# Last chunk of tokens kept in its own order and stored by SyncE; the first 1024 tokens sorted by themselves and gathered by index

## What is computed

```python
x   = local + block-summary attention(q, k, v)          # (1536, 512), 8 heads of 64
xn, en = x / |x|, expert_emb / |expert_emb|
logits = xn @ en.T / tau;  e = argmax(logits);  gate = softmax(logits)[e]
y[t]   = gate[t] * (relu(x[t] @ w1[e[t]]) @ w2[e[t]])   # 8 experts, 512 -> 1024 -> 512
h   = y @ w_in                                          # 512 -> 2048
g   = (a0 + a1 h + a2 h^2 + a3 h^3) / (1 + |b0||h| + |b1| h^2 + 1e-6)
out = g @ w_out                                         # 2048 -> 512, row t of out is token t
```

## Time and profile before

| | |
|---|---|
| median of 3 runs | 752.04 us |
| profiled execution | 747.03 us |
| its span, first to last instruction | 745.5 us |
| TensorE busy | 684.3 us (92%) |
| VectorE busy | 500.2 us (67%) |
| ScalarE busy | 419.7 us (56%) |
| GpSimd busy | 171.9 us (23%) |
| mean granted TensorE clock | 0.970 |

### The profile page before, as it was taken

The page is one execution under the profiler, slowest core; times in us unless marked ns, Lnnn a source line. Parts: engine busy times, 40 slices in busy tenths (PEclk is TensorE's granted clock), DMA queues, the critical chain, the costliest instruction groups (busy, mean ns, idle before and its releaser), DMA issues.

```text
span 745.5 us, 11775 instructions
## 1 busy us (share of the span) xinstructions
PE 684.3 (92%) x3397; PEld 547.3 (73%) x3397; DVE 500.2 (67%) x975; ACT 419.7 (56%) x786; POOL 171.9 (23%) x233
## 2 busy tenths in 40 slices
PE   4769999999387989999999999999999999999991
PEld 4457777777276777777888788888888888888871
DVE  7576677676557468433411637899989899898881
ACT  5445565565335577533523527777666666766650
POOL 4366999331331312111001000100000020200002
PEclk9989999999599999999999999999999999999997
DMA  8233544311698499823723440101000020100001
GB/s 295 56 93 113 135 131 109 79 47 45 212 325 252 139 308 323 276 59 105 265 84 100 142 157 15 57 0 30 15 14 1 1 71 1 42 15 1 0 1 56
DMA packets 52182, 77.75 MB, mean 104 GB/s; under 512 B 31680, under 2 KB 31696, under 8 KB 50840
## 3 DMA queue, kind: packets, MB, share of 16 engines
q1 hardware_dynamic: 43608, 51.51, 22.4%
q0 software_dynamic: 8064, 25.46, 10.3%
q10 hardware_dynamic: 448, 0.02, 0.1%
HBM read 63.50 MB, written 13.48 MB: 103 GB/s over the span
## 4 chain that ended last, share of the span: by engine, by line
PE 76%; DMA 10%; DVE 5%; ACT 3%; issue 2%; SPq 1%; POOL 1%; DVEq 1%; ACTq 0%; POOLq 0%
PE bank L1594 18%; PE bank L1609 17%; PE bank L1562 10%; PE bank L1341 10%; PE bank L1541 8%; DMA raw_late<-in_moe_w_dram 8%; PE bank L1450 4%; PE bank L1424 4%; PE bank L1449 3%; DVE weights L1206 2%; ACT weights L792 2%; DMA kraw<-in_k_dram 2%; PE bank L1469 1%; PE bank L1357 1%; DMA x_by_slot<-VA,zidx 1%
## 5 line engine op out<-in xcount | busy, mean ns | idle before, releaser
L1609 PE MATMUL bank<-weights,G 128*128 128x512 f32 x576 | 140.7, 393 | 1.9 <-DVE G L1206 1.9
L1594 PE MATMUL bank<-X2T,weights 128*128 128x512 f32 x576 | 141.1, 394 | 0.0
L1609 PEld LDWEIGHTS bank<-weights,G 128*128 128x128 f32 x576 | 108.1, 188 | 27.1 <-DVE G L1206 2.6
L1594 PEld LDWEIGHTS bank<-X2T,weights 128*128 128x128 f32 x576 | 107.5, 188 | 23.6
L1541 PE MATMUL bank<-weights,XT 128*128 (+1 forms) x456 | 116.9, 406 | 8.2 <-issue 4.0
L1562 PE MATMUL bank<-weights,HT 128*128 x456 | 112.6, 403 | 6.0 <-DVE HT L1206 6.0
L1541 PEld LDWEIGHTS bank<-weights,XT 128*128 128x128 f32 x456 | 85.3, 192 | 30.4 <-issue 11.8
L1562 PEld LDWEIGHTS bank<-weights,HT 128*128 128x128 f32 x456 | 85.7, 191 | 26.4 <-issue 7.1
L844 ACT ACTIVATE qd<-bank,coef 128x512 f32<-128x512 f32 x48 | 33.1, 689 | 73.5 <-PE bank L1594 73.4
L1206 DVE TENSOR_TENSOR HT<-bank,HT 128x512 fp32r<-128x512 f32 x38 | 24.5, 685 | 70.2 <-ACT HT L869 68.5
L742 ACT ACTIVATE es<-es,nmx 128x182 f32<-128x182 f32 x96 | 42.5, 444 | 25.5 <-DVE nmx L1015 25.5
(11 more groups left out here) (215 smaller groups left out, 1156.1 us busy)
## 6 DMA issues: line engine op xcount, KB each, us to landing
raw_early<-in_moe_w_dram SPq DMA_DIRECT2D x14, 1024.0 KB, 8.2
raw_late<-in_moe_w_dram SPq DMA_DIRECT2D x14, 1024.0 KB, 10.3
y_in_order<-yo POOLq DMA_DIRECT2D x19, 256.0 KB, 3.2
x_all<-in_moe_w_dram POOLq DMA_DIRECT2D x8, 512.0 KB, 3.9
kraw<-in_k_dram SPq DMA_DIRECT2D x3, 1024.0 KB, 8.3
qraw<-in_q_dram SPq DMA_DIRECT2D x12, 256.0 KB, 4.1
x<-y_in_order POOLq DMA_DIRECT2D x12, 256.0 KB, 3.1
VA<-in_v_dram SPq DMA_DIRECT2D x10, 208.0 KB
```

What stands on the lines that cost most here:

```text
L1594: last = T_.matmul(bank[6 + f % 2][:, :], W[:, 0, wa, kc * F2 + f * P:kc * F2 + (f + 1) * P], X2T[c % 2][:, xa, kc * C_TOK:(kc + 1) * C_TO ...
L1609: last = T_.matmul(bank[tt][:, :], G[:, f % 2, ga, tt * P:(tt + 1) * P], W[:, 1, wa, f * DM:(f + 1) * DM], start=(f == 0 and n_ == 0), sto ...
```

## The change

Only the first 1024 tokens (8 tiles, `SORTED`) take part in the sorting for stage C. The rows of `y_in_order` stay where they are. A second index `s_at` tells a token's place when only those 1024 are sorted by expert; the scatter of gates (now three values: gate, token, row in `y_in_order`) goes by `s_at` and has 8 parts instead of 12. Every tile of stage C is now gathered with an indirect DMA: the first 8 by `y_row` (read back with the gates), the last 4 by `c_at`, which leaves these 512 tokens in their own order. So the last chunk is gated from `gate_id` directly, and its four output tiles are stored by SyncE with direct DMAs. Chunk 0 is loaded later (in tile 14 and 15), gated in tile 16, three of its tiles are transposed in tile 17 ahead of `g2`, and the fourth (kept in `xg[0]`) behind that `g2`, its halves made at the start of `tile_b(18)`. GpSimd now stores chunk 0 before it loads the last tile.

```diff
@@ TensorE
+                if T == SORTED:
+                    last = T_.matmul(b_[:, at + E:at + 2 * E], ones[:, :], seen[:, T % 2, :], start=True, stop=True)
@@ x2_transposes
-                if T == CT:
+                if T == 2:
                     pe.wait_ge(bx_lo, MAXT)
+                elif T == CT - 1:
+                    pe.wait_ge(cx_lo, 1)
+                elif T == CT:
+                    pe.wait_ge(cx_lo, CT - 1)
@@ tile_b, TensorE
-                for tt in FIRST_X2.get(i, ()):
-                    x2_transposes(0, tt)
+                if i == MAXT - 2:
+                    for tt in range(CT - 1):
+                        x2_transposes(0, tt)
                 if ahead == 0:
                     c1(0)
                     c1(1)
                 g2(i, par, e)
+                if i == MAXT - 2:
+                    x2_transposes(0, CT - 1)
@@ tile_b, ScalarE (VectorE likewise: x2_lo behind its three register loads)
                 act.wait_ge(g2_mm, i + 1)
+                if i == MAXT - 1:
+                    x2_hi(0, CT - 1)
...
-                for tt in FIRST_X2.get(i, ()):
-                    x2_hi(0, tt)
+                if i == MAXT - 2:
+                    for tt in range(CT - 1):
+                        x2_hi(0, tt)
@@ tile_b, VectorE
+                if i == MAXT - 3:
+                    for T in range(CT):
+                        gated(T)
@@ places, VectorE
-                V.tensor_copy(c_at[:, :], top1[:, :]).then_inc(c_at_ready, 1)
+                link(V.tensor_copy(c_at[:, :], top1[:, :]))
+                link(V.tensor_copy(gate_id[:, :, 2], top1[:, :]))
+                link(V.scalar_tensor_tensor(early_count[:, :], iota_e[:, 0, :], -float(REGION), early_count[:, :], ALU.mult, ALU.add))
+                pre = thr[:, :, 0:E]
+                link(V.tensor_tensor(pre, tri[:, :, :], early_count[:, :].unsqueeze(1).to_broadcast([P, E, E]), ALU.mult))
+                link(V.tensor_reduce(shift, pre, AX.X, ALU.add))
+                link(V.tensor_tensor(shift, shift, early_count[:, :], ALU.subtract))
+                link(V.tensor_tensor(shift, before, shift, ALU.subtract))
+                part = [P, SORTED, E]
+                link(V.tensor_tensor(LG2[:, 0:SORTED, :], oh[:, 0:SORTED, :], shift.unsqueeze(1).to_broadcast(part), ALU.mult))
+                link(V.tensor_reduce(first[:, 0:SORTED], LG2[:, 0:SORTED, :], AX.X, ALU.add))
+                link(V.tensor_tensor(first[:, 0:SORTED], top1[:, 0:SORTED], first[:, 0:SORTED], ALU.subtract))
+                V.tensor_copy(s_at[:, :], first[:, 0:SORTED]).then_inc(c_at_ready, 1)
@@ load_x2, GpSimd
-                if T >= X2_SLOTS:
-                    pool.wait_ge(cx_mm, T - X2_SLOTS + 1)
-                pool.dma_start(x2[:, T % X2_SLOTS, :], ys[T * P:(T + 1) * P, :]).then_inc(x2_in[T % X2_SLOTS], 16)
+                if T == CT - 1:
+                    pool.wait_ge(bx_mm, MAXT)
+                elif T >= CT:
+                    pool.wait_ge(cx_mm, T - CT + 1 if T < CT + X2_SLOTS else T - X2_SLOTS + 1)
+                where = y_row[:, T:T + 1] if T < SORTED else c_at[:, T:T + 1]
+                G_.indirect_dma_start(out=x2_tile(T), out_offset=None, in_=ys[0:2 * C_TOK if T < CT else N, :],
+                                      in_offset=bass.IndirectOffsetOnAxis(ap=where, axis=0))\
+                  .then_inc(x2_extra if T == CT - 1 else x2_in[T if T < CT else (T - CT) % X2_SLOTS], 16)
@@ the tile loop, GpSimd
-                if i == tiles_for(0) + 1:
+                if i == MAXT - 5:
+                    pool.wait_ge(token_ready, 1)
+                    pool.wait_ge(y_out, 16 * (MAXT - 4))
                     for T in range(X2_SLOTS):
                         load_x2(T)
                 if i == MAXT - 4:
-                    load_x2(X2_SLOTS)
+                    load_x2(CT - 1)
@@ SyncE, at its end
+            for T in range(SORTED, NT):
+                sp.wait_ge((acc_dve, acc_act)[T % 2], T // 2 + 3)
+                sp.dma_start(out[T * P:(T + 1) * P, :], ost[:, T % CT, :]).then_inc(last_out, 16)
+            sp.wait_ge(last_out, 16 * CT)
```

More of the change, by code:

```diff
@@ L162, in moe_mlp_kernel @@
         zidx = ra.take("zidx", [P, E], U32)
+        early_count = ra.take("early_count", [P, E], F32)
         upper = ra.take("upper", [P, P], BF16)
@@ L343, in rank_bank, with x2_bank, x2_tile, wait_x2 @@
             return 6 if T == NT - 2 else 7
-        def tiles_for(c):
-            return min(MAXT, (c + 1) * CT + E - 1)
-        def x2_bank(c, tt):
-            return (6 if c == 0 else 4) + tt % 2
+        def x2_bank(T):
+            return (6, 7, 4, 6)[T] if T < CT else 4 + T % 2
+        def x2_tile(T):
+            if T < X2_SLOTS:
+                return x2[:, T, :]
+            return xg[0] if T == CT - 1 else x2[:, (T - CT) % X2_SLOTS, :]
+        def wait_x2(eng, T):
+            if T == CT - 1:
+                eng.wait_ge(x2_extra, 16)
+            elif T < X2_SLOTS:
+                eng.wait_ge(x2_in[T], 16)
+            else:
+                eng.wait_ge(x2_in[(T - CT) % X2_SLOTS], 16 * ((T - CT) // X2_SLOTS + 2))
         def halves_of(f):
@@ L1284, in tile_b @@
                 other = dve.value_load(other_of[0:1, i:i + 1], min_val=0, max_val=1)
+                if i == MAXT - 1:
+                    x2_lo(0, CT - 1)
                 for half in range(2):
@@ L1297, in tile_b @@
                     x_lo(i + 2)
-                for tt in FIRST_X2.get(i, ()):
-                    x2_lo(0, tt)
-                for tt in FIRST_X2.get(i + 1, ()):
-                    gated(tt)
+                if i == MAXT - 2:
+                    for tt in range(CT - 1):
+                        x2_lo(0, tt)
                 with dve.If(new):
```

55 lines of the change are left out of this document (32 added, 23 removed).

## The result

The changed kernel takes 745.76 us (median of 15 runs, 739.67 to 749.86), the kernel before 750.56 us in 15 runs beside it (744.59 to 752.91). The ratio is 0.9935, with a 95% interval of 0.991 to 0.9961: faster by 0.4 to 0.9%, where 754.8 us and slower was predicted.

A forecast was written before the change was run, and what follows sets the result against it. TensorE was taken to bound the kernel from about 320 to 727 us, with weight loads before and the last stores after. Terms 2.2 + 0.5 + 2.2 - 2.1 = +2.8 us on 752.04 gave 754.8 us, range 751.8 to 758.2.

The forecast's parts named there:

- Term 4: End of the kernel: SyncE issuing the last stores instead of GpSimd gains 2.1 us (0.3 to 3.3).
- rival 4: End: it shrinks by more than the stores, by 0 to 8.1 us of possible GpSimd queue wind-down; chance 0.08.
- rival 1: Weight loads take up the delay of `places()`, so terms 1 and 2 vanish: 752.1 us; chance 0.12.
- term 1: `places()` on VectorE: ten added instructions delay `g2` of tile 1 and the following weight loads by 2.2 us.
- Term 2: `g2` of tile 1: TensorE's longer wait lowers its clock, costing 0.5 us (0 to 2.0).
- Term 3: Passage from stage B to C: `c1(0)` waits for VectorE's `x2_lo` of the fourth tile, 2.2 us (1.7 to 2.2).
- The alternative that the prediction named: Passage: if VectorE's register loads took no longer than ScalarE's 1.07 us, ScalarE decides and the delay is 1.7 us.
- Edits at nothing: Other edits, such as fewer gate scatters and gathers for direct loads, cost nothing; tile 18's x load keeps 12 us of cover.
- Rival 2: Passage: the clock also falls behind TensorE's new wait ahead of `c1(0)`, 1.5 us more, 756.3 us; chance 0.2.
- Rival 3: Fourth tile's late gather holds VectorE in `gated` when hidden tile 17 needs it: about 1 us, 755.8 us; chance 0.1.

The follow-up runs named there:

- e1: The kernel before with its last four output tiles stored by SyncE in sorted order; ratio 0.9881, 737.12 us beside 746.85.
- e2: The changed kernel with its four direct last stores issued by GpSimd instead of SyncE; ratio to the kernel before 1.0051.
- e5: The changed kernel with one more small GpSimd transfer behind the last copy, waited for; single execution, 752.91 us.
- e9: The changed kernel with one more small GpSimd transfer some 5 us ahead of the last copy's end; single execution, 742.91 us.
- e13: The changed kernel run again unchanged; ratio to the kernel before 0.9894.
- e14: The changed kernel with gate scatter rows of two values instead of three, token number as the gathers' index; ratio to the kernel before 0.9926.
- e19: The changed kernel run again unchanged, beside other kernels on another chip; ratio to the kernel before 0.9935.
- e4: The changed kernel with `s_at` made at the end of tile 1 and the gate scatters in tiles 1 to 4; ratio to the kernel before 0.9916.
- e7: The changed kernel with late `s_at`, tile 18's x load ahead of the gathers, and fourth-tile transposes inside `g2` of tile 17; ratio 0.9837, 736.02 us.
- e12: The kernel before run again unchanged; single execution, 747.7 us.
- e16: The kernel before with 128 bytes a partition of padding ahead of `token_of`; ratio 1.0012.
- e17: The kernel before with 96 bytes a partition of padding ahead of `token_of`; ratio 1.0021.
- e11: The kernel before with gate scatter rows of three values (12 bytes) instead of two; single execution, 743.88 us.
- e15: The kernel before with gate scatter rows of 12 bytes instead of 8, timed; ratio 0.9928, 744.82 us beside 748.96.
- e3: The changed kernel with GpSimd's load of x for tile 18 ahead of the three gathers, which move to the next tile; ratio to the kernel before 0.9936.
- e10: The kernel before with its last four gate scatters moved from tiles 4 and 5 to tiles 8 and 9; ratio 0.9985.
- e8: The changed kernel with the four omitted gate scatters put back in tiles 4 and 5, into an unread tensor; ratio to the kernel before 0.9913.
- e18: The changed kernel with gate scatter rows of 8 bytes and twelve scatters, four into an unread tensor; ratio to the kernel before 0.9952.

## Why the prediction was wrong

**Term 4, the end: the step that failed.** The prediction compared the landings of the last stores (737.4 and 735.3 us) and let the 8.1 us between landing and end of span stay, since "all engines stand idle there alike". That part is there: SyncE's last store lands 2.2 us after its issue, at 743.4 + 2.2 = 745.6, which is 2.2 us behind the copy against 4.8 before (737.3 - 732.5): 2.6 us gained where 2.1 was predicted, within its 0.3 to 3.3. The rest, 10.4 - 2.6 = 7.8 us, is rival 4, which had a chance of 0.08: what follows GpSimd's last landing. The step that failed is that these 8.1 us were put at nothing as common to both kernels, while 7.67 us of them are GpSimd's own closing DRAIN. e1 and e2 show that they go and come with the engine that issues, e5 and e9 that they count from GpSimd's own last transfer and run beside other work, and the DRAIN of after is over at 672.9 us. The price lay at its upper end, for GpSimd's last store of after was issued 84 us ahead of the end. The argument against it was no argument: that all engines are idle in a stretch tells what they don't do, not what the program waits for. Nor was it so that no row explains the 8.1 us: the view of line 74 of before has it. Without that row they should have entered the range as a bound of the term; the change touched exactly what ended ahead of them.

Two smaller things of the same sum: its base, 752.04 us, was a median of three runs, and that of 15 is 750.56; and the lower edge of the range, 751.8 us, does not follow from its own bounds, which with rival 1 give 752.04 + 1.7 - 3.3 = 750.4.

The Trainium skill, "DMA: Bandwidth & Descriptors", section "Anatomy of one DMA — SWDGE (gpsimd) path", speaks of the fixed cost of one transfer; the 2.0 and 2.4 us that were estimated by that page are near the 2.6 us that the landings gained, and tell nothing of the other 7.8 us.

**Terms 1 and 2, `places()` and the clock: right in place and about right in size, but not seen in the total.** `s_at` ends 2.25 us after `c_at` (238.91 and 236.66, term 1 had 2.2), TensorE waits 4.46 us as forecast, `g2` of tile 1 begins 2.25 us later behind M (36.95 - 34.70), and takes 8.19 us; the granted clock there:

```profile
241.00:250.00 9.00, 8.27 (x26) 6.58 (x27) 6.16 (x5) 3.28 (x3) 1.58 (x2) 0.67 0.38 37
```

It is 0.67, and was 0.76 in the earlier trace rows. The larger clock term (8.19 - 7.41 = 0.8, not 0.5) is within its bounds. Over the ten traces with `places()` as it is, `g2` of tile 1 begins 36.7 to 37.4 us behind M, against 34.6 to 34.9 in the kernel before and its variants, so term 1 is in all of them. Term 2 is in seven (8.0 to 8.3 us); in e13, e14 and e19 the clock had fallen one wait earlier and `g2` took 5.9. e4, which takes both terms away, has the stretch 3.6 us shorter than after and 1.2 shorter than e13 and e19; that is one trace, and its ratio overlaps that of the changed kernel. Rival 1, that the weight loads take up the delay, fits that the stretch is not longer than before; against it, e4 and e7 (146.2 and 146.9 us) lie below all ten traces with the delay. Those are two traces, and the times don't decide. What was missed is that the stretch from M to tile 11 differs from execution to execution of kernels of one kind by more than the terms: 148.2 to 155.8 us in the five traces of the kernel before and its kin (before, e1, e12, e16, e17; mean 151.3), 147.4 to 151.9 in the ten of the changed kernel with `places()` as it is (mean 149.9), 145.7 to 146.9 in e11, e15, e4 and e7.

**Term 3, the passage: right.** The wait ahead of `c1(0)` is for `x2_lo`, 1.76 us; with the load of x out of the way (e3) the stretch is 41.78 - 39.77 = 2.0 us longer, within 1.7 to 2.2. The step that was off is VectorE's register loads: the chain runs through ScalarE's `yo`, its own loads (up to 463.66) and its `x2_hi`, and VectorE follows at once. The alternative that the prediction named was the true one.

**Edits at nothing: one was wrong.** The load of x for tile 18 was said to have 12 us of cover: 18.0 us between issue and use (435.09 - 417.13) less 6 for the store's landing and the gathers. That left out the load's own landing, and took 2.8 us for the store's, the median of the output scatters. The trace of before has this very store and this very load, beside the first two loads of `w_out` (DMA issues of 415.5 to 425 us: size, us from issue to landing):

```profile
y_in_order<-yo POOLq DMA_DIRECT2D x1, 256.0 KB, 7.4
xg<-x_by_slot POOLq DMA_DIRECT2D x1, 256.0 KB, 6.8
```

The store is issued 1.1 us ahead of the load there, and lands 6.3 us behind its issue. With that, three gathers of 1.26 us and 6.8 us for the load, 18.0 - 6.3 - 3.8 - 6.8 = 1.1 us of cover are left, by numbers that were there to read. In after the store took longer and two gathers took 2.36 and 1.88 us, and TensorE waited 3.56. So it went in four of ten traces, at up to 5.3 us each (47.09 - 41.78), the wait and the clock behind it, as in term 2; in e4 the clock did not fall behind it (3.37 us, then 5.85 for the products).

**Rival 2, the clock at the passage: seen in one trace of the eleven with the wait** (7.42 instead of 5.88 us, e13). The row of before on which the argument against it stood was one draw of two: ahead of the last 12 products TensorE waits 1.8 to 1.9 us in all 20 traces, and they take 3.0 to 3.1 us in twelve, among them before and after, and 4.2 to 4.6 us in eight (e4, e5, e10, e11, e12, e14, e15, e17). **Rival 3**, a late gather of the fourth tile: in no trace did `c1(0)` wait for anything but the halves. The last gather of the four, issued at 441.71 in after, was early enough.

The Trainium skill, "TensorE: Matmul & The Clock Gate", section "Part 1: The HAM clock gate (the "warmup" mystery)", says that the moment at which the clock changes varies from run to run (it says it of the rise). Here a fall behind one and the same wait comes or doesn't: 7.42 us for the products in e13 against 5.88 in e3, behind 1.75 and 1.76 us of wait.

**The sum as measured.** -10.4 at the end, +2.0 at the passage, +0.7 for the SBUF layout, +2.2 for the load of x (the mean of ten traces), and for the stretch of the weight loads the difference of the two means above, 149.9 - 151.3 = -1.4: -6.9 us. The medians give 745.76 - 750.56 = -4.8 us, the interval -6.8 to -2.9. The sum lies at its edge, and the term that can carry the rest is the weight loads, whose means rest on five and ten traces that scatter by several us. The forecast of +2.8 us was 7.6 us too high, about the 7.8 of the closing DRAIN; that the load of x (+2.2) and the weight loads, with whatever offset terms 1 and 2, cancel in the rest is luck.

**What stays open.** Why the stretch of the weight loads isn't longer than before by the 3 us of terms 1 and 2. Rows of 12 bytes in the scatters of gates make the kernel before faster (e15, its interval excludes 1); the layout doesn't (e16, e17), fewer scatters beside the loads gave no gain in time though the loads landed faster (e10), and in the changed kernel neither going back to 8 bytes nor to twelve scatters takes anything away that can be measured (e14, e8, e18). Row size is thus shown as a cause in one kernel and not in the other, and how it acts on the loads isn't shown at all.

## What to carry to other kernels

When the end of a span seems to have no row, look for the instruction that closes each engine's program: in these kernels GpSimd's takes 7.7 to 8.1 us behind its last landing, and letting another engine issue the last few transfers moves it beside the last products. A load that is moved behind other entries of a queue is to be costed with the landings of its own stretch, beside the large transfers that run there, and not with the median over the kernel, and its own landing belongs to the cost. And where two profiled executions agree in their spans, go through them stage by stage before saying that nothing happened.

## What the runs showed of the hardware

- GpSimd's closing DRAIN took 7.67 to 8.08 us in 20 traces, VectorE's 0.73, ScalarE's 0.6, SyncE's 0.12 and less. Where GpSimd has the last transfer, the span ends 10.8 to 11.7 us after its issue, for 256 KB by index or direct and for a small transfer alike (ten traces); with SyncE's direct stores last, 2.4 to 2.7 us after the last copy (ten traces).
- A direct store of 256 KB by GpSimd kept it waiting for 8.0 us behind two loads of 1 MB, against a median landing of 3.4 (in the kernel before it landed in 7.4 us there, and the load of x in 6.8); GpSimd's indirect issues took 1.01, 2.36 and 1.88 us there, against 0.96.
- A shift of tiles in SBUF by some bytes changed 270 us of products and element work by 0.7 us, from 273.98 in each of four traces to 274.7 in each of fifteen (e13 has 276.3, with its slower products at the passage), and the 63.3 us from tile 11 to 16 to 62.5 in e11, e15 and e16 (a shift of 128 bytes), but not in e17 or in the changed kernel (96 bytes).
- Behind a wait of one length the clock falls in some executions and not in others: 1.8 to 1.9 us ahead of the last 12 products, 3.0 to 3.1 us for them in twelve traces, 4.2 to 4.6 in eight. Ahead of `g2` of tile 1, waits of 2.25 to 2.65 us were followed by a fall in the eight traces in which the 12 products ahead had run at the full clock (7.3 to 7.4 us for 24), and a wait of 2.9 us by none in the three in which those had run slow (5.9 us).
- Scattering rows of 12 bytes instead of 8 beside the weight loads gave 0.9928 (0.9899 to 0.9957).
